# A shorter chain to the loop's flag, a flag read one double sooner, and three moves of side work, in a fused attention and mixture-of-experts kernel on one core

## The reference, cut to what matters

```python
# u, v: (8, 3072, 256), z: (8, 3072, 64), float32
scores = z @ z.transpose(0, 2, 1) / S           # per batch, S = 3072
attn = np.maximum(scores, 0.0) ** 2
x = (u * (attn @ v)).reshape(B * S, D)          # 24576 rows of 256
logits = x @ w_gate                             # E = 8 experts, top 1
gate_w = softmax(logits)[argmax]
for i in range(N):                              # in the order of the rows
    e = expert_idx[i]
    if counts[e] < capacity:                    # capacity = 3072 // 8 * 2 = 768
        disp[e, counts[e]] = x[i]; pos[i] = counts[e]; counts[e] += 1; keep[i] = True
y = relu(disp @ w1) @ w2                        # per expert, F = 1024
out[i] = gate_w[i] * y[expert_idx[i], pos[i]] if keep[i] else 0
```

## Time and profile before

| what | value |
|---|---|
| median of 3 runs | 869.93 us (869.71 to 869.93) |
| the profiled execution: its time, its span | 869.84 us, 868.1 us |
| granted TensorE clock, mean | 0.999 of full speed |
| busy: PE, DVE, ACT, POOL | 98%, 73%, 66%, 14% |
| share of the chain of waits: PE, DVE, issue | 93%, 2%, 2% |
| group n = 17, first matmul to first matmul | 563.08 to 594.86 us |
| first scores matmul of n = 10 | 339.74 us |
| first absolute sum of n = 17 | 563.41 us |
| a tile's transpose into `xT`, issue to landing, median | 2.4 us |
| the flag of n = 17 written by VectorE | 577.05 us (0.14 us long) |
| TensorE's first expert matmul, L775 | 612.54 us |

### The profile page before, as it was taken

How to read it: one execution, slowest core, us unless ns; L and a number is a source line. 1 busy time by engine, 2 the same in 40 slices (tenths; PEclk the granted TensorE clock), 3 DMA queues, 4 the chain that set the end, 5 groups by cost and what they waited for, 6 DMA issues and landing times.

```text
span 868.1 us, 22767 instructions
## 1 busy us (share of the span) xinstructions
PE 854.4 (98%) x7257; PEld 684.0 (79%) x7258; DVE 632.7 (73%) x1380; ACT 574.6 (66%) x874; POOL 121.5 (14%) x121
## 2 busy tenths in 40 slices
PE   6999999999999999999999999999999999999997
PEld 5888888888888887888888888888677777777776
DVE  7976877988888988788888798687465655565531
ACT  6978786868778679787778777678344434435422
POOL 0001101101101110110110110110112121211212
PEclk9999999999999999999999999999999999999999
DMA  7923254354323662432442441721725325315101
GB/s 288 352 74 112 68 164 155 83 167 136 106 75 115 232 165 76 139 93 63 134 108 55 127 134 44 273 72 36 129 83 171 84 92 163 136 52 151 55 18 36
DMA packets 127797, 104.52 MB, mean 120 GB/s; under 512 B 90669, under 2 KB 115322, under 8 KB 126752
## 3 DMA queue, kind: packets, MB, share of 16 engines
q1 hardware_dynamic: 122880, 91.61, 35.7%
q0 software_dynamic: 4896, 12.64, 4.1%
HBM read 40.03 MB, written 44.93 MB: 98 GB/s over the span
## 4 chain that ended last, share of the span: by engine, by line
PE 93%; DVE 2%; issue 2%; ACT 1%; DMA 1%; SPq 1%; ACTq 0%; POOL 0%; DVEq 0%; POOLq 0%
PE O L664 16%; PE O L668 16%; PE O L666 16%; PE Sc L775 14%; PE Sc L629 8%; PE Sc L630 8%; PE O L798 3%; PE O L800 3%; PE O L802 3%; PE M L798 2%; PE M L800 2%; PE M L802 2%; PE M L705 1%; ACT Sc L451 0%; DMA x<-disp 0%
## 5 line engine op out<-in xcount | busy, mean ns | idle before, releaser
L664 PE MATMUL O<-vS,attn_hi 128*128 128x256 f16 x1332 | 363.0, 273 | 1.3 <-DVE vS L917 1.2
L668 PE MATMUL O<-vS,attn_lo 128*128 128x256 f16 x1332 | 363.0, 273 | 0.0
L666 PE MATMUL O<-vS,attn_hi 128*128 128x256 f16 x1332 | 363.0, 273 | 0.0
L451 ACT ACTIVATE Sc<-Sc 128x768 f32<-128x768 f32 x224 | 178.0, 795 | 87.8 <-PE Sc L630 79.0
L934 DVE TENSOR_TENSOR attn_lo<-attn,attn_hi 128x768 f16<-128x768 f32 x223 | 213.7, 958 | 7.7
L455 ACT ACTIVATE attn<-Sc 128x768 f32<-128x768 f32 x224 | 181.8, 811 | 7.1
L664 PEld LDWEIGHTS O<-vS,attn_hi 128*128 128x128 f16 x1332 | 130.3, 98 | 28.8 <-issue 1.4
L666 PEld LDWEIGHTS O<-vS,attn_hi 128*128 128x128 f16 x1332 | 130.3, 98 | 26.4
L629 PE MATMUL Sc<-zP 128*128 (+1 forms) x450 | 146.5, 326 | 1.6 <-DVE zP L900 0.9
L630 PE MATMUL Sc<-zQ,zP 128*128 (+1 forms) x450 | 146.4, 326 | 0.0
L928 DVE CAST attn_hi<-attn 128x768 f16<-128x768 f32 x223 | 123.7, 555 | 30.2 <-ACT attn L455 26.2
(11 more groups left out here) (155 smaller groups left out, 911.6 us busy)
## 6 DMA issues: line engine op xcount, KB each, us to landing
out<-empty SPq DMA_DIRECT2D x16, 1536.0 KB, 6.4
wraw<-in_moe_w SPq DMA_DIRECT2D x16, 1024.0 KB
rawv<-in_v SPq DMA_DIRECT2D x14, 768.0 KB, 7.7
ubuf<-in_u SPq DMA_DIRECT2D x19, 384.0 KB, 3.2
disp<-vS SPq DMA_DIRECT2D x8, 774.0 KB, 8.8
rawz<-in_z SPq DMA_DIRECT2D x3, 768.0 KB
xT<-xrow SPq DMA_TRANSPOSE x54, 2.4
disp<-xrow,slot POOLq DMA_INDIRECT x54
```

The costliest lines, as they stand in the source:

```text
L451: act.activation(pair, pair, ACT.Relu).then_inc(s["relu_done"], 1)
L664: nc.tensor.matmul(o_part(t), hi, v[:, 0:D], start=c == 0 and j == 0 and t % 2 == 0, stop=False, skip_group_check=True)
L666: nc.tensor.matmul(o_part(t), hi, v[:, D:2 * D], start=False, stop=False, skip_group_check=True)
L668: ins = nc.tensor.matmul(o_part(t), lo, v[:, 0:D], start=False, stop=c == PAIRS - 1 and j == 1, skip_group_check=True)
```

## The change

1. **Start.** `onesb` and `ones` are filled before the other tables. `base` loses its second half and `over` becomes `room`; `first_z(2)` sums v's parts (L946 before) between its subtraction and its two copies.
2. **Head of a group.** ScalarE writes `rows_hi` in double 0, right behind the absolute sums and ahead of its next relu. VectorE computes `lbits`, `rinv`, `rscale` ahead of the low half of double 1 (which used to come first), then `rows_lo`, `rowfac`, and only then the halves of double 2.
3. **Routing.** Logits follow the first tile of double 3, not the last. VectorE makes the high half of double 5 between `onehot` and the counts, which TensorE now puts in the middle of a scores quartet (`between`); its low half follows the slots. The flag comes from `room`, a running sum of counts less capacity, reduced right behind `posf`, with a semaphore of its own (`least_ready`). The four instructions that end in `xrow`'s gate weight come after the low half.
4. **Flag.** `END_AT` = 4: all engines read the flag after the fifth double.
5. **Weights.** The maxima of expert 0 lie in n = 8 and 9, of expert 1 in n = 9, 10 and 11; scales in n = 9. GpSimd's reductions go to n = 9 and 12.
6. **SyncE.** The transpose of `x0` no longer waits for u's load in its queue, and takes the due count that the group before wrote.

Cut to its core:

```diff
@@ start, VectorE
+            dve.memset(onesb[:, :], 1.0)
+            dve.memset(ones[:, :], 1.0).then_inc(consts, 1)
             for e in range(E):
                 dve.memset(rank[:, :, e:e + 1], float(E - e))
...
-            dve.memset(onesb[:, :], 1.0)
-            dve.memset(ones[:, :], 1.0).then_inc(consts, 1)
+            def sum_v():
...
+            first_z(2, sum_v)
@@ ScalarE
-                        if not peeled and c == ROWS_HI_AT:
                             act.wait_ge(s["rscale_ready"], n)
                             for t in range(TILES):
                                 act.activation(halves[:, t, 0:D], ubuf[:, t, :], ACT.Copy, scale=rscale[:, t:t + 1]
@@ TensorE
-            def scores(K, n, c, par):
+            def scores(K, n, c, par, between=None):
...
+                    if between is not None and j == 0:
+                        between()
...
-                                scores(K0 + c + LEAD, n, c + LEAD, par)
+                                scores(K0 + c + LEAD, n, c + LEAD, par, count if c == COUNTS_AT and not peeled else None)
@@ VectorE, head of a group
+                            do_lo(K0 + 1, 1)
                             for t in range(TILES):
                                 dve.wait_ge(s["rows_hi"], (n - 1) * TILES + t + 1)
...
-                        do_hi(K0 + c + 2, c + 2)
-                        do_lo(K0 + c + 2, c + 2)
+                        if peeled or c != ROUTE_AT:
+                            do_hi(K0 + c + 2, c + 2)
+                            if c < PAIRS - 1:
+                                do_lo(K0 + c + 2, c + 2)
@@ VectorE, routing
+                            do_hi(K0 + c + 2, c + 2)
+                            dve.wait_ge(s["counts_ready"], n)
...
+                            route(dve.tensor_tensor(room[:, :], room[:, :], M[1][:, TILES * E:(TILES + 1) * E], ALU.add))
+                            route(dve.tensor_tensor(posf[:, :, :], counts, over_tiles(base[:, :]), ALU.add))
+                            dve.tensor_reduce(least[:, :], room[:, :], AX.X, ALU.min).then_inc(s["least_ready"], 1)
+                            route(dve.tensor_tensor(fullp[:, :, :], posf[:, :, :], over_tiles(limit[:, :]), ALU.is_ge))
+                            dve.wait_ge(s["least_ready"], n)
+                            dve.tensor_scalar(ends[0:1, bass.ds((n - 1) & (NG - 1), 1)], least[0:1, :],
+                                              0.0, float(NG + 1), ALU.is_lt, ALU.mult
+                                              ).then_inc(s["flag_ready"], 1)
@@ SyncE
-                wait_apart(sp, s["loaded_u"], n * 16 + 16)
...
-                    wait_apart(sp, s["scattered"], sp.snap(due))
+                    wait_apart(sp, s["scattered"], sp.snap(due) + 48)
...
+                    wait_apart(sp, s["loaded_u"], n * 16 + 16)
@@ GpSimd
-                    only_if(pool, n == 8, lambda: all_w(0))
-                    only_if(pool, n == 9, lambda: all_w(1))
+                    only_if(pool, n == 9, lambda: all_w(0))
+                    only_if(pool, n == 12, lambda: all_w(1))
@@ the table of places
-W_MAX_AT = (6, 7, 8, 9)
-W_SCALES_AT = 10
+W_MAX_IN = (((8, 7), (8, 8), (8, 9), (9, 6)), ((9, 7), (9, 9), (10, 9), (11, 6)))
+W_SCALES_IN = (9, 8)
...
-LOGITS_AT = (3, 2)
-COUNTS_AT = (4, 1)
+LOGITS_AT = (3, 0)
+COUNTS_AT = 4
...
-END_AT = 5
+END_AT = 4
+DUE_AT = 5
```

More of the change, by code:

```diff
@@ L670, in weigh, with count @@
                     return ins
+                def count():
+                    pe.wait_ge(s["onehot_ready"], n)
+                    counts = M[1][:, 0:(TILES + 1) * E].rearrange("p (t e) -> p t e", t=TILES + 1)
+                    nc.tensor.matmul(M[1][:, 0:(TILES + 1) * E], before[:, :],
+                                     onehot[:, :, :].rearrange("p t e -> p (t e)"), start=True, stop=False,
+                                     skip_group_check=True)
+                    for k in range(TILES):
+                        ins = nc.tensor.matmul(counts[:, k + 1:TILES + 1, :], ones[:, :],
+                                               onehot[:, k:k + 1, :].to_broadcast([P, TILES - k, E]),
+                                               start=False, stop=k == TILES - 1, skip_group_check=True)
+                    ins.then_inc(s["counts_ready"], 1)
                 def part(start, stop):
@@ L708, in part @@
                                 ins.then_inc(s["logits_ready"], 1)
[L709 to L717, removed]
-                                                           onehot[:, k:k + 1, :].to_broadcast([P, TILES - k, E]),
-                                                           start=False, stop=k == TILES - 1, skip_group_check=True)
-                                ins.then_inc(s["counts_ready"], 1)
                         if peeled and c == 0:
@@ L911, in first_z @@
                 z_lo(to, h, col)
+                if between is not None:
+                    between()
                 dve.tensor_copy(hi_across[out, to:to + SLICE * P], hi[own, to:to + SLICE * P]).then_inc(s["khi_ready"], 2)
@@ L1068, in part @@
                             first_v(2 + V0_AT.index(c))
-                        if not peeled and c == ROUTE_AT[0]:
+                        if not peeled and c == ROUTE_AT:
                             dve.wait_ge(s["logits_ready"], n)
@@ new lines, in part @@
+                            assert rs[0] == ROUTE_STEPS, rs[0]
+                        if not peeled and c == DUE_AT:
+                            dve.tensor_scalar(lacking[:, :], base[0:1, 0:1], float(GROUP), 48.0, ALU.is_lt, ALU.mult
+                                              ).then_inc(s["due_ready"], 1)
+                            dve.wait_ge(s["due_ready"], n * 2 + 1)
+                            dve.scalar_tensor_tensor(out=dues[0:1, bass.ds(n & (NG - 1), 1)],
+                                                     in0=xrow[0:1, 0, D + 1:D + 2].bitcast(I32), scalar=48.0 / GROUP,
+                                                     in1=lacking[:, :], op0=ALU.mult, op1=ALU.add
+                                                     ).then_inc(s["due_ready"], 1)
```

96 lines of the change are left out of this document (35 added, 61 removed).

## The result

The changed kernel took 879.56 us (median of 4 runs, 879.11 to 879.84) against 869.93 (869.71 to 869.96): slower, ratio 1.0111, 95% interval 1.0093 to 1.0128. The forecast was 872.2 (869.8 to 874.6): the sign was right, the size was not. The profiled execution took 879.45, span 877.7 against 868.1.

A forecast was written before the change was run, and what follows sets the result against it. The prediction took TensorE's instructions to bound the loop, with none removed. From 869.84 us: start -1.0, head +1.6, flag +2.2, n = 1 +0.2, weights +1.1, end -1.8, giving 872.2 (range 869.8 to 874.6).

The forecast's parts named there:

- The way from a written flag to TensorE's branch is 1.06: Behind the flag (F, its write's end): next matmul at F + 1.17 to 1.20, stall 0.12 to 0.15 in 17 groups, +2.2.
- Head of a group: Before double 2's weighing: its low half comes late, TensorE stalls 0.08 to 0.10 in every group, +1.6 in all.
- Slack of over 1 us: In the kernel before, TensorE's flag reader came a double later and had over 1 us to spare.
- Flag chain: Routing on VectorE: from first logits matmul (L) to flag written (F) takes 3.28 us, 0.37 less than before.
- The overlap of two VectorE instructions: In the flag chain, `least` and `fullp` overlap as traced; the skill's rule would make the flag 0.1 to 0.2 later.
- n = 1: First group: its first flag read is slower, +0.2, besides the head and flag stalls of every group.
- logits that wait for a transpose: At the logits: a sign that would refute the forecast, which had the last transpose in time by 0.3.
- Weights: Groups 3 and 9 to 12: late low halves and an extra maximum cost more than spreading saves, +1.1, bounds 0 and 2.5.
- Start: Before the loop: `ones` 0.35 and `vscale` 0.66 sooner, -1.0 together; -0.6 if only one counts.
- End: From the last group to L775: flag 1.6 sooner, way out 0.2 shorter with VectorE's drain late, -1.8.
- Sum: Whole kernel: all terms together give +2.3 on the profiled 869.84, so 872.2.

The follow-up runs named there:

- e2: The kernel before, with only SyncE's wait for u's load put behind x0's transpose and the piece of zeros: 872.13 us, ratio 1.0026.
- e5: The changed kernel with the piece of zeros at the head of SyncE's group in n = 10 to 16, behind SyncE's flag up to n = 9: 875.95 us.
- e6: e5 with the third `rows_lo` and `rowfac` moved behind double 2's halves at a group's head: 873.57 us, ratio 1.0043.
- e7: e6 with a shorter chain to the flag (fewer waits) and the gate weight's steps woven into the slots' chain: 868.61 us, ratio 0.9985.
- e8: e7 with the weights' maxima, scales and GpSimd's reductions at the places of the kernel before: 868.41 us, ratio 0.9985.
- e3: e1 with `END_AT` = 5, so the flag is read after the sixth double again: 874.44 us, ratio 1.0051.
- e1: The changed kernel with SyncE's piece of zeros issued behind the wait for u's load again: 878.98 us, ratio 1.0098.
- e12: e8 run again unchanged, beside e11 on the same chip: 868.94 us, ratio 0.9991.
- e11: e8 with ten more filling matmuls (66, not 56) on TensorE at the start: 868.76 us, ratio 0.9987.
- e9: e8 with ScalarE's two conversions of expert 0's first weights in n = 9 two doubles sooner: 870.10 us, ratio 1.0001.

## Why the prediction was wrong, point by point

- **The step that failed** is "The way from a written flag to TensorE's branch is 1.06", used for all 17 groups. It holds in nine, and in n = 1 but for the slower first read that has a term of its own. In the changed kernel's n = 9 to 15 the load inside it takes 0.92 and not 0.31, and the stall is 0.72 to 0.79, not 0.12: 5.26 - 7 x 0.115 = 4.5 us. The load is long while the piece of zeros is being written: SyncE issued it 0.9 to 1.4 after the flag before and 0.7 to 0.9 ahead of it now. I had followed SyncE's move for the transposes and for x0, and left out the one other DMA that it issues behind them. Timelines of SyncE, before in n = 13 (flag out at 449.98):

```profile
449.06 1.47 SPq L308 DMA_TRANSPOSE x<-disp  x1
450.91 0.62 SPq L312 DMA_DIRECT2D out<-empty  x1
```

and after (flag out at 456.33):

```profile
453.76 1.46 SPq L309 DMA_TRANSPOSE x<-disp  x1
455.58 0.62 SPq L313 DMA_DIRECT2D out<-empty  x1
```

  TensorE's load stands at F + 0.48 to F + 0.8 when it is short. e2 shows the load's length to hang on SyncE's order alone, e5 that taking the DMA away restores it in place. In groups 2 to 8 and in n = 16 SyncE is late with its other work (the piece goes out 10 to 14 us behind TensorE's load), and in n = 17 there is no piece: so the seven. Why a write in flight makes a load longer, no run shows.

  The trace of the kernel before had it already, on the engines that read the flag after the piece had gone out, GpSimd in n = 9 to 15 and SyncE itself in n = 1 to 8:

```profile
L231 POOLq TENSOR_LOAD <-ends x7: 373/872/922, 323.8 to 515.9; - x7
L231 SPq TENSOR_LOAD <-ends x8: 862/880/905, 77.9 to 306.2; - x8
```

  There the piece went out only 0.3 to 0.9 us after TensorE's load had begun. The prediction read this way in n = 17 alone, a group without a piece.

  Without the long loads (e5) the kernel takes 875.95, which is still above the range: the terms below make up the rest.
- **Head of a group.** Forecast 0.08 to 0.10, measured 0.10 to 0.12 in the plain groups; e6 took it away by the order that the reasoning pointed to.
- **Slack of before.** "Slack of over 1 us" was wrong too, as e2 shows (0.3); it changed no term. With the flag read after the sixth double, two register instructions and two waits of TensorE's sequencer for the keys stand between its branch and the next scores, some 0.5 us more than after the fifth. In the kernel before, n = 17 (its branch is at 578.2, the next scores at 579.17):

```profile
L207 PEldq EVENT_SEMAPHORE  x2: 51/51/51, 578.5 to 578.6; - x2
```

- **Flag chain.** Forecast F = L + 3.28, measured 3.27 in all groups but the first; stall 0.12 to 0.15 forecast, 0.10 to 0.16 measured in n = 2 to 8, 16 and 17. e7 shows that 0.24 less of chain ends it. The overlap of two VectorE instructions, which the sum took from the row and not from the rule, holds: the chain came out at 3.27.
- **n = 1.** Forecast +0.2 and the share of every group, 0.4; measured +1.07. The transposed tiles were not in time for the sooner logits there (0.57), which I had checked on n = 17 alone: logits that wait for a transpose were one of the signs that I had named for a wrong forecast. The long first load cost 0.54.
- **Weights.** Forecast +1.1. In n = 10 the low half of double 1 was 0.70 late (0.65 forecast), in n = 12 the evacuation 0.81 and what follows 0.22 (0.5 to 0.7 forecast), in n = 9 0.48 stayed at double 11 of the 0.59: the term was short by about 0.6. e8 shows that the new places are not to blame once VectorE has its slack back.
- **Start.** Forecast -1.0, measured -0.07 at the first scores of double 3 and -0.20 a group later. I compared `vscale` with ScalarE's end at 16.73 and had 0.15 of margin, from one execution; v landed 0.9 later in the changed kernel's (12.07 against 11.13 at ScalarE's third sum). With v at 11.04, in e8's, the start is 1.03 sooner. In late ones TensorE, whose filling matmuls now end 0.6 sooner, can idle long enough to lose its clock.
- **End.** Forecast -1.8, measured -1.88, with VectorE's drain last, as written, and L779 3.25 after the flag (3.4 forecast). The expert phase lost 0.54 at one wait that I had not looked for.
- **Sum.** Forecast +2.3. Short by 4.5 (load), 0.8 to 0.9 (start), 0.7 (n = 1), 0.5 (expert phase), 0.6 (weights), and 0.2 spread over n = 2 to 8.

## What to carry to other kernels

When a wait is moved in the program of the queue engine, list every DMA behind it and where each will be in flight, not only the one that the move is for. A sequencer's load of a register lies on TensorE's path at each data-dependent branch; here it was three times as long under a large transfer, so such a branch wants either slack of 0.6 us or a quiet moment. A margin of 0.1 to 0.2 us against a DMA's landing, read from one execution, is no margin.

## What the runs showed of the hardware

- A load of one word into a register took 0.30 to 0.33 us on TensorE and VectorE and 0.28 to 0.29 on ScalarE, 0.49 to 0.57 in the first use on these three, and 0.86 to 0.97 on TensorE when the piece of zeros (1.5 MB) had been issued 1.1 to 2.8 us before it (the changed kernel, e2, e3); with 1.0 to 1.2 us between them (e1) it took 0.45 to 0.90. TensorE's matmuls kept their 0.109 under the same write.
- TensorE idle for 1.78, 1.94 and 1.58 us by its rows at the start (the changed kernel, e12, e11) kept the granted clock at 1.00. Idle for 2.06, 2.22 and 2.18 us (e1, e7, e9) it went on to 3.4 us at 0.50, in e7 from 1.3 us after it had started again, and the first whole group began 1.5 to 1.7 us later than in the changed kernel.
- The third piece of v reached ScalarE between 11.0 and 12.5 us in the 14 traces. Why is open: the issues of those DMAs stand at the same times to within 0.1 us. Open is also what made the late wait in the expert phase of the changed kernel, e1 and e5, and not of e3 and e6.
